# The first six steps in an order written out per engine, four of them on unrounded weights

## The reference, cut to what matters

```python
mask = (rel >= 0) & (rel < 64)                 # 4 batches, 8 heads, 576 positions, head size 64
attn = softmax(where(mask, scale * q @ k.T, -1e9)); x = attn @ v
h = x @ w_in                                   # (2304, 512) @ (512, 2048)
sp = np.where(h > 20.0, h, np.log1p(np.exp(np.minimum(h, 20.0))))
g = h * np.tanh(sp)
x = g @ w_out                                  # (2304, 2048) @ (2048, 512)
...
out[do_compute] = xc + y                       # y: the chosen expert of 8, by gate and row
```

## Time and profile before

| what | value |
|---|---|
| three runs | 742.6, 747.21, 749.05 us (median 747.21) |
| the profiled execution | 745.0 us; its span 743.4 us |
| mean granted TensorE clock of it | 0.977 |
| PE busy | 692.1 us, 93% of the span |
| DVE, ACT, POOL busy | 497.3 (67%), 360.7 (49%), 273.0 us (37%) |
| PE busy from 130 to 600 us | 463.65 of 470 us |
| PE busy from 0 to 10, 10 to 20, 20 to 30 us | 2.24, 6.64, 7.65 us |
| PE busy from 40 to 50, 50 to 60, 60 to 70, 80 to 90 us | 4.69, 7.87, 8.06, 6.57 us |
| granted clock from 40 to 50, 50 to 60, 60 to 70, 90 to 100 us | 0.83, 0.83, 0.53, 0.83 |

### The profile page before, as it was taken

The page is one execution under the profiler, slowest core; times in us unless marked ns, Lnnn a source line. Parts: engine busy times, 40 slices in busy tenths (PEclk is TensorE's granted clock), DMA queues, the critical chain, the costliest instruction groups (busy, mean ns, idle before and its releaser), DMA issues. The chain is left out here.

```text
span 743.4 us, 13820 instructions
## 1 busy us (share of the span) xinstructions
PE 692.1 (93%) x4974; PEld 615.4 (83%) x4974; DVE 497.3 (67%) x930; ACT 360.7 (49%) x789; POOL 273.0 (37%) x239
## 2 busy tenths in 40 slices
PE   4877799999999999999999999998999978999993
PEld 3766689988888988988988988987988968999892
DVE  3647985786686686686687677679588626455360
ACT  4445655555555555455455555553544215343430
POOL 4235524344344334434335335245543321121221
PEclk9987999999999999999999999999999989999998
DMA  9524113116117214214214123102647689999940
GB/s 270 174 92 150 36 41 97 36 36 120 45 36 141 80 36 97 69 36 93 61 47 93 47 61 94 36 1 55 229 149 257 190 294 392 348 344 357 348 136 2
DMA packets 62834, 97.16 MB, mean 131 GB/s; under 512 B 23014, under 2 KB 27110, under 8 KB 62768
## 3 DMA queue, kind: packets, MB, share of 16 engines
q1 hardware_dynamic: 59280, 91.27, 39.9%
q0 software_dynamic: 3168, 4.51, 1.9%
q10 hardware_dynamic: 320, 0.52, 0.3%
HBM read 84.97 MB, written 13.73 MB: 133 GB/s over the span
## 5 line engine op out<-in xcount | busy, mean ns | idle before, releaser
L1393 POOL TENSOR_TENSOR q_sb<-n_sb,r_sb 128x512 f32<-128x512 f32 x72 | 93.2, 1294 | 298.0 <-DVE u_sb L1040 187.9
L588 PE MATMUL Y<-wout_hi,g_hi 128*128 128x512 f32 x288 | 120.0, 417 | 11.8 <-ACT g_hi L815 11.7
L588 PE MATMUL Y<-wout_lo,g_hi 128*128 128x512 f32 x288 | 115.4, 401 | 0.0
L569 PE MATMUL H<-x_hi,win_hi 128*128 128x256 f32 x384 | 113.1, 295 | 0.9 <-DVE x_lo L981 0.9
L569 PE MATMUL H<-x_hi,win_lo 128*128 128x256 f32 x384 | 109.9, 286 | 0.0
L569 PE MATMUL H<-x_lo,win_hi 128*128 128x256 f32 x384 | 109.9, 286 | 0.0
L1399 POOL TENSOR_TENSOR g_lo<-g_sb,g_hi 128x512 fp32r<-128x512 f32 x72 | 95.3, 1323 | 0.8
L675 PEld LDWEIGHTS H<-xT,w 128*128 128x128 f32 x768 | 90.0, 196 | 5.5 <-DMA w<-moe_w 4.6
L675 PE MATMUL H<-xT,w 128*128 128x128 f32 x768 | 90.6, 280 | 4.2 <-DMA w<-moe_w 4.2
L1025 DVE TENSOR_SCALAR u_sb<-e_sb 128x512 f32<-128x512 f32 x72 | 37.2, 517 | 79.3 <-ACT e_sb L800 78.7
L588 PE MATMUL Y<-wout_hi,g_lo 128*128 128x512 f32 x288 | 81.6, 406 | 6.2 <-POOL g_lo L1399 6.1
(11 more groups left out here) (194 smaller groups left out, 1398.6 us busy)
## 6 DMA issues: line engine op xcount, KB each, us to landing
w<-moe_w SPq DMA_DIRECT2D x24, 2048.0 KB, 10.3
kT<-k_T SPq DMA_DIRECT2D x32, 256.0 KB, 3.1
vw<-v_w SPq DMA_DIRECT2D x32, 256.0 KB, 3.2
y_rows<-ytile SPq DMA_DIRECT2D x36, 128.2 KB
out_rows<-ytile SPq DMA_DIRECT2D x36, 128.0 KB
win<-moe_w_in SPq DMA_DIRECT2D x8, 512.0 KB, 8.6
qbd<-q_T SPq DMA_DIRECT2D x64, 64.0 KB, 2.5
wout<-moe_w_out SPq DMA_DIRECT2D x8, 512.0 KB, 8.1
```

What stands on the lines that cost most here:

```text
L569: last = nc.tensor.matmul(HM3[J % 3][:, f, :], wt[:, j, d, f * P:(f + 1) * P], xt[:, c % 2, d, :], start=(n == 0), stop=(n == 3 * DB - 1))
L588: last = nc.tensor.matmul(Y[t][:, :], gt[:, J % 2, lo:lo + P], wt[:, 2 * j + f, :], start=(j == 0 and f == 0 and wt is wout_hi and gt is g ...
L1393: nc.gpsimd.tensor_tensor(q_sb[:, :], n_sb[:, J % 2, :], r_sb[:, J % 2, :], ALU.mult).then_inc(q_ok, 1)
```

## The change

It does this:

- The preamble of every engine now covers steps 0 to 5 in an order of its own (`OPENING = 6`), and `tick` runs from J = 6. `mish_g` is cut into `mish_a`, `mish_b` and `mish_c`, with a buffer `a_sb` of their own, so that they can stand apart.
- Steps 0 to 3 (`RAW = 4`) use `down_raw`: g is written unrounded to `g_raw` (in the memory of `g_hi`) and multiplied by the unrounded W_out slice as loaded, 4 matmuls of 128x128 by 512 columns in fp32 in place of 12 in fp32r. These steps have no `g_hi_out` and no `g_lo_out`. Slices 1, 3, 5 and 7 are rounded and split in steps 7 to 10 instead, for their use from step 8 on.
- POOL makes no lo part any more. It rounds slices 0, 2, 4, 6, 8; ACT the other eleven; all sixteen lo parts are on DVE.
- The first chunk's PE order has four score groups ahead of the transposes. Its loads are shared by two queues: SP issues q and k of batches 0 and 2 and v of 2 and 3, ACT the others. SP's list of slices is rearranged; slice 12 now stands ahead of group 6.

```diff
+        RAW = 4
+        OPENING = 6
...
             def down(J):
                 c, j = divmod(J, NJ)
-                pe.wait_ge(ghi_ok, J + 1)
-                if c == 0:
+                pe.wait_ge(ghi_ok, J + 1 - RAW)
+                if j == 0:
+                    pe.wait_ge(y_ok, c)
+                if c == 0 or late_slice(J - 1):
                     slice_split(pe, 2 * j + 1)
-                elif j == 0:
-                    pe.wait_ge(y_ok, c)
...
+            def down_raw(J):
+
+                pe.wait_ge(g_ok, J + 1)
+                pe.wait_ge(slice_in[2 * J + 1], 16)
+                if J == 0:
+                    pe.wait_ge(pT_ok, NB)
+                for t in range(TT):
+                    for f in range(2):
+                        lo = f * CT + t * P
+                        last = nc.tensor.matmul(Y[t][:, :], g_raw[:, J % 2, lo:lo + P], wout[:, 2 * J + f, :],
+                                                start=(J == 0 and f == 0), stop=False)
+                last.then_inc(g2_ok, 1)
...
+            weigh_v(1, 0)
+            scores(1, 1)
+            up(2)
+            down_raw(0)
+            probs_T(1, 1)
+            up(3)
+            scores(1, 2)
+            down_raw(1)
+            weigh_v(1, 1)
+            up(4)
+            probs_T(1, 2)
+            up(5)
+            weigh_v(1, 2)
+            down_raw(2)
+            scores(1, 3)
+            down_raw(3)
+            up(6)
+            probs_T(1, 3)
+            up(7)
+            scores(2, 0)
+            down(4)
+            weigh_v(1, 3)
+            down(5)
+            for J in range(OPENING, NC * NJ):
                 tick(J)
...
+        def late_slice(J):
+
+            return 2 * (J - NJ + 1) + 1 if NJ - 1 <= J < NJ - 1 + RAW else None
...
-                if J < len(HI_TICKS):
-                    for s in HI_TICKS[J]:
-                        round_slice(s)
+                if late_slice(J):
+                    round_slice(late_slice(J))
```

More of the change, by code:

```diff
@@ L143, in build @@
         yT1 = q_sb[:, :].rearrange("p (d t) -> p d t", d=DB)
+        with ExitStack() as raw_g:
+            g_raw = sb("g_raw", [P, 2, 512], FP32, raw_g)
         g_hi = sb("g_hi", [P, 2, 512], F32R)
@@ L384, in _ @@
             sp.sem_inc(placed, 2)
-            for b in range(NB):
-                load_first(b)
+            load_first(0)
+            load_first(2)
+            for b in (2, 3):
+                sp.dma_start(v0[0:W, b, :], v_in[b, W:2 * W, :]).then_inc(v0_in[b], 16)
             load_slice(0)
@@ L629, in tick @@
                 gs, gp = scores_at(J), probs_at(J)
-                if gs and not gp and J > 1:
+                if gs:
                     scores(*gs)
@@ L637, in tick @@
                     rows_T(0, 0, 0)
[L638 to L641, removed]
+                if gp:
                     probs_T(*gp)
@@ L646, in tick @@
                 down(J)
-                if gp and J > 0:
+                if gp:
                     weigh_v(*gp)
-                if J == 0:
-                    probs_T(*gp)
                 if t in (0, 1):
@@ L866, in tick @@
                 ahead = J + 1 < NC * NJ
-                if ahead and J > 0:
+                if ahead:
                     mish_exp(J + 1)
[L869 to L872, removed]
                 if gp:
@@ L924, in _ @@
             mish_exp(1)
-            round_slice(3)
-            for J in range(NC * NJ):
+            round_slice(10)
+            x_hi_out(1, 0)
+            mish_recip(1)
+            round_slice(12)
+            att_exp(1, 1)
+            mish_exp(2)
+            round_slice(14)
+            probs_T_out(1, 1)
+            mish_recip(2)
+            mish_exp(3)
+            att_exp(1, 2)
+            x_hi_out(1, 1)
+            mish_recip(3)
+            mish_exp(4)
+            probs_T_out(1, 2)
+            round_slice(9)
+            round_slice(11)
+            mish_exp(5)
+            mish_recip(4)
+            round_slice(13)
+            round_slice(15)
+            x_hi_out(1, 2)
+            att_exp(1, 3)
+            mish_recip(5)
+            g_hi_out(4)
+            mish_exp(6)
+            probs_T_out(1, 3)
+            mish_recip(6)
+            g_hi_out(5)
+            x_hi_out(1, 3)
+            for J in range(OPENING, NC * NJ):
                 tick(J)
@@ L986, in rest_of_slice @@
                     dve.wait_ge(slice_in[s], 16)
+                if s % 2 and s // 2 < RAW:
+                    dve.wait_ge(g2_ok, s // 2 + 1)
                 nc.vector.tensor_tensor(of_slice(s, win_lo, wout_lo), of_slice(s, win, wout),
@@ L1199, in tick @@
                     logits_out(c - 1, 0)
-                if gp and J > 0:
+                if gp:
                     normalise(*gp)
                 mish_g(J)
-                if J == 0:
-                    soften(*scores_at(-1))
-                    normalise(*gp)
                 if route_at(c, j) == 2:
@@ L1470, in _ @@
             mish_q(0)
-            rest_of_slice(3)
-            for J in range(NC * NJ):
+            mish_q(1)
+            mish_q(2)
+            mish_q(3)
+            mish_q(4)
+            mish_q(5)
+            g_lo_out(4)
+            mish_q(6)
+            g_lo_out(5)
+            for J in range(OPENING, NC * NJ):
                 tick(J)
```

171 lines of the change are left out of this document (103 added, 68 removed).

## The result

The changed kernel takes 722.62 us (median of 4 runs, 720.04 to 726.11) against 747.62 us of the kernel before beside it (4 runs): ratio 0.9677, 95% interval 0.9639 to 0.9715. Run again in a later group it took 721.21 us (median of five executions; a sixth, in a slower state, took 729.35 and is left out) against 743.38, ratio 0.970 (0.9669 to 0.9732). So it is 22 to 25 us faster; forecast were 16. The profiled execution took 722.84 us, its span 721.3.

What follows compares the result with a forecast made beforehand. PE was taken as the bound, losing time to waits and low clock in the opening: up(8) 16.7 us earlier, less 1.5 for late splits, is 15.2 us off, 732.0 against the 747.2 median, stated as 731; range 722 to 742.

Steps and rivals of the forecast that it cites:

- The bound and the mark: PE loses 25.7 us to waits and low clock between first matmuls of up(0) and up(8); up(8) marks the gain.
- the best end: Whole kernel with no contention and no late cost: 722 us.
- Start of up(0): First chunk: scores ahead of transposes and two loading queues bring the last x_lo at 22.9, not 27.7: 4.9 us gained.
- Down_raw: Steps 0 to 3: an unrounded down takes 3.75 us, 1.0 more than a rounded one; PE pays 4 us.
- Up(0): First up on PE: at the pace of the 1.2 GHz level it takes 5.28 us, 2.4 too many.
- Contention and low clock: Opening: seven q and two g_lo on POOL slow DVE, 4 us, plus 1 us low clock; up(8) at 85.2.
- the walk: Stepping through all five engines' lists in the opening: PE waits 2.6 us together, up(8) at 80.2 before contention.
- The waits that stay: PE in the opening still waits for c(0) and the normalises of (1,2), 0.9, and (1,3), 0.5: together 2.6 us.
- The input slices: Slices 9 and 11 land near 56 and 57.5; c of step 3 at 60.4, covered by 1 us: no cost.
- Late splits: Steps 7 to 10: an extra ACT rounding and DVE split each, mostly covered; 1.5 us, 9 if laid bare.
- DVE as the bound: Rival for the opening: all nine contentions paid plus low clock, up(8) near 93, kernel 740 us; chance 0.12.
- Slower by a low clock: Rival: PE stays at the low clock level through the opening; about 775 us if throughout; chance 0.06.

Runs made afterwards that it cites:

- late splits doubled: The changed kernel with rounding done twice on ACT and two more DVE subtractions in each of steps 7 to 10: 729.6 us, ratio 0.9816 to the kernel before.
- busy POOL: The changed kernel with 12 more subtractions of 128x512 on POOL, two behind each of q(0) to q(5): 729.45 us, ratio 0.9806 to the kernel before.
- x_hi of batch 3 first: The changed kernel with x_hi of batch 3 ahead of the exps of group (1,0) on ACT: 721.78 us, ratio 0.9712 to the kernel before.

## Why the prediction was right, and where it was not

**The bound and the mark** were right: PE lost its time between up(0) and up(8), and what up(8) gained is what the kernel gained. Span less up(8) is 641.5 us before and 643.5 after. Of the 2.0 us, 0.8 are the late splits; the rest is not explained, and kernels of this set differ by more there (638.6 to 643.6, the one with late splits doubled left aside).

**The size** was too small: 16 us forecast, 22 to 25 measured. 722.62 us lies just above the best end, 722, and just below the 723 to 738 to which the forecast gave 0.66. Up(8) was put at 85.2 and came at 77.83, below the 83 to 88 named; up(0) and the distance of two down_raw matmuls lie below their marks too. By terms:

- *Start of up(0)*, forecast 22.9, came at 21.66: 1.2 us.
- *Down_raw*, 3.75 forecast, 3.54 measured: 0.8 us over four. I scaled the expert stage's 0.236 us for 128 columns; with 512 columns a matmul takes 0.885, which is 0.221 for 128. The lower end was taken as 3.71 from four times a rounded matmul, and the truth is below that too: 3.8 times, not four.
- *Up(0)* took 4.34 us (21.66 to 26.00), not 5.28: 0.9 us. That was luck of the execution: in the repeat it took 5.28 us, and started 0.7 earlier.
- *Contention and low clock*, 5 us forecast. This is the step that failed. DVE's instructions were lengthened as forecast: over the opening by some 5.8 us (0.75, 1.07, 1.07, 1.08, 0.95 and three of 0.4 or less, each row's duration less that of its kind alone; the 0.75 beside a rounding on POOL that was not among the nine). But PE's waits stayed at 2.7 us, what the walk gave without any contention. I had added DVE's loss to PE's path after having found 9 us of gaps on DVE, 43 us of work in 52. The busy POOL shows that the cover ends: the next 12 cost 0.7 to 0.8 us each. The 1 us of low clock behind these waits did not come either.
- These make 7.9 of 7.4; the rest is 0.5 us more of small pieces on PE.

**The waits that stay** were right in size (2.6 forecast) and in place: 1.29 us for g_raw(0) (1.1 forecast), 0.43 for the normalise of (1,2), 0.74 for that of (1,3), 0.19 for c(3). **The input slices** landed as forecast: c(3) behind slices 9 and 11 ended at 59.4 (60.4 forecast). The 1 us of cover was not there, since PE too was earlier: it waited 0.19 us. In other kernels with the same list that place cost 1.82 us (x_hi of batch 3 first), and 2.11 us and the clock (late splits doubled). **Late splits** were put at 1.5 and cost 0.8.

**The rivals.** DVE as the bound did not come, but is near. Slower by a low clock did not come: from the end of up(0) to 130 us the granted clock of the change is 1.00 throughout. Its mechanism is real: low stretches stand behind waits of 2.11, 2.41 and 2.44 us. But a wait of 2.26 us had none behind it, so the length alone does not decide. The 775 us for PE at the low level throughout is loose: 49 us more for 49 us of work make 779, and at the 2.4 on 2.92 of up(0) 770.

The rule of the Trainium skill (GPSIMD Engine Reference, Specifications), as the prediction told it, agrees with the trace in part. Splits and an a with two SBUF inputs were slowed, and c, which reads PSUM, was not (0.68 at 34.53). But two a that began some 0.05 us ahead of a q kept their 0.69 us (at 29.52 and 42.77), and u, with one SBUF input, went from 0.43 to 1.50. The sentence gives no size, and by exposure alone the sum would have been worse still. As to the clock, the page TensorE: Matmul & The Clock Gate of the Trainium skill (What's actually happening) says that activity releases the throttle. The trace agrees between these two kernels: from 22 to 78 us the change has PE busy 53.20 us and clock 0.97, the kernel before 44.99 us and 0.85. With POOL kept busy 48.26 us of work had 0.97 as well.

**What I did not see** is why PE waited for g_lo before: q(1) stood ahead of g_lo(0) on POOL. I took the 4.6 us out of the sum with the instructions, so the number was right without the reason. Nor did I say which part of the change earns how much. The runs give most of it to the unrounded downs with what moves with them (15 us alone), 5 to 6 to the first chunk, and 2 to 3, not shown to differ from none, to the written-out order of the steps once these two are there.

## What to carry to other kernels

Before an order is rewritten, look in each engine's list for the instruction on the critical path that stands behind another step's waiting one; leaving out the conversions that stand there for the first few steps and moving the splits that served them behind the opening, at the price of slower matmuls, gained here as much as reordering everything (728.63 and 729.13 us). A slowdown of an engine that has gaps is charged to those gaps first, and only the part beyond them to the path. That gaps take up the first part is read from the rows here, that the rest is paid is shown by the busy POOL. An earlier start is worth nothing if the next wait grows by as much, and a grown wait can cost nearly its length again in TensorE's clock (1.70 us behind waits of 2.11, 2.41 and 2.44 us, nothing behind one of 2.26).

## What was not expected of the hardware

- Unrounded fp32 matmuls of 512 columns take 0.885 us each in a row at granted clock 1.00, 3.8 times the 0.232 of a rounded one.
- A POOL product of two SBUF operands (q, 1.26 us alone) made three of DVE's instructions beside it 1.07 or 1.08 us longer whatever their own length: 0.43 to 1.50, 0.69 to 1.77, 1.22 to 2.29. All three began after the q and ended as if they had waited for its end; others beside a q or g_lo were 0.25 to 0.95 us longer, or not at all.
- Waits of PE of 2.11, 2.41 and 2.44 us were followed by down_raw at 5.40 us in place of 3.70; those of 1.29, 1.82 and 2.26 were not. What decides it besides the length was not tried.
